# Reordered opening loads and first-chunk work in a fused attention and expert kernel

## The reference

```
B, H, S, D = 4, 8, 768, 48
for t in range(S):                                   # attention, per batch and head
    cur = einsum('bhd,bhe->bhde', u * k_t, v_t)
    y_t = einsum('bhd,bhde->bhe', r_t, state + cur)
    state = w * state + einsum('bhd,bhe->bhde', k_t, v_t)
x = y as (3072, 384)                                 # tokens x model width
h = maximum(maximum(x @ w1, x @ w2), x @ w3);  x = h @ w_out        # 384 -> 768 -> 384
logits = x @ w_gate + log1p(exp(x @ w_noise)) * noise               # 8 experts, best two
out[token] += weight * (maximum(x @ w1[e], 0) @ w2[e])              # 384 -> 1024 -> 384
```

## Time and profile before

| | before |
|---|---|
| median of 3 runs | 884.25 us |
| profiled execution | 883.62 us |
| its span | 881.7 us |
| TensorE (PE) matmul busy | 865.3 us, 98% |
| VectorE (DVE) busy | 450.2 us, 51% |
| ScalarE (ACT) busy | 270.8 us, 31% |
| GpSimd (POOL) busy | 391.4 us, 44% |

### The profile page before, as it was taken

The page is one execution under the profiler, slowest core; times in us unless marked ns, Lnnn a source line. Parts: engine busy times, 40 slices in busy tenths (PEclk is TensorE's granted clock), DMA queues, the critical chain, the costliest instruction groups (busy, mean ns, idle before and its releaser), DMA issues. The chain is left out here.

```text
span 881.7 us, 19581 instructions
## 1 busy us (share of the span) xinstructions
PE 865.3 (98%) x6562; PEld 846.8 (96%) x6563; DVE 450.2 (51%) x1100; ACT 270.8 (31%) x520; POOL 391.4 (44%) x380
## 2 busy tenths in 40 slices
PE   6999999999999999999999999999999999999996
PEld 5999999999999999999999999999999999999996
DVE  7674646546464655637574563452525335264322
ACT  4441323223231322225315342421414243143210
POOL 5254325343352544234454556453534426455442
PEclk9999999999999999999999999999999999999999
DMA  9795112222221211031115622615325252432221
GB/s 227 176 301 135 46 42 65 64 62 52 61 57 47 66 54 38 2 135 55 46 46 191 196 58 65 182 54 166 97 66 180 79 181 73 151 123 70 64 79 52
DMA packets 103765, 86.08 MB, mean 98 GB/s; under 512 B 60634, under 2 KB 93090, under 8 KB 103696
## 3 DMA queue, kind: packets, MB, share of 16 engines
q1 hardware_dynamic: 82704, 31.56, 15.1%
q10 hardware_dynamic: 8576, 27.33, 9.6%
q0 software_dynamic: 12416, 26.28, 9.5%
HBM read 70.46 MB, written 21.35 MB: 104 GB/s over the span
## 5 line engine op out<-in xcount | busy, mean ns | idle before, releaser
L1413 PE MATMUL ps<-yh,wh 128*128 128x384 f32 x432 | 148.2, 343 | 1.6 <-DVE wl L715 0.6
L1304 ACT ACTIVATE gh<-ps 128x384 fp32r<-128x384 f32 x136 | 66.9, 492 | 264.6 <-PE ps L1415 264.6
L1415 PE MATMUL ps<-yh,wl 128*128 128x384 f32 x432 | 145.1, 336 | 0.0
L1413 PE MATMUL ps<-xgh,w1h 128*128 128x384 f32 (+1 forms) x456 | 145.0, 318 | 0.0
L1414 PE MATMUL ps<-yl,wh 128*128 128x384 f32 x432 | 145.0, 336 | 0.0
L1415 PE MATMUL ps<-xgh,w1l 128*128 128x384 f32 (+1 forms) x456 | 145.0, 318 | 0.0
L1414 PE MATMUL ps<-xgl,w1h 128*128 128x384 f32 (+1 forms) x456 | 145.0, 318 | 0.0
L1060 DVE SCALAR_TENSOR_TENSOR gl<-ps,gh 128x384 fp32r<-128x384 f32 x136 | 75.8, 557 | 126.8 <-ACT gh L1304 126.8
L1413 PE MATMUL ps<-w2h,gh 128*128 128x384 f32 x408 | 138.2, 339 | 0.6 <-DVE gl L1054 0.6
L1414 PE MATMUL ps<-w2l,gh 128*128 128x384 f32 x408 | 136.6, 335 | 0.0
L1415 PE MATMUL ps<-w2h,gl 128*128 128x384 f32 x408 | 136.5, 335 | 0.0
(11 more groups left out here) (202 smaller groups left out, 1484.2 us busy)
## 6 DMA issues: line engine op xcount, KB each, us to landing
ew_raw<-ew ACTq DMA_DIRECT2D x28, 768.0 KB, 4.6
v_sb<-vN SPq DMA_DIRECT2D x24, 192.0 KB, 3.1
out<-zrow SPq DMA_DIRECT2D x1, 4608.0 KB, 15.9
x_rows<-x_sb ACTq DMA_DIRECT2D x8, 576.0 KB, 3.8
kn_sb<-kN SPq DMA_DIRECT2D x20, 192.0 KB, 2.9
k_raw<-kT SPq DMA_DIRECT2D x48, 72.0 KB, 2.3
wraw<-moe_w SPq DMA_DIRECT2D x6, 576.0 KB, 7.5
e_raw<-ew SPq DMA_DIRECT2D x4, 768.0 KB, 4.3
```

The source lines that it names most:

```text
L1304: act.activation(gh[:, f, :], ps[f % 4][:, 0:T], ACT.Relu).then_inc(gh_ok, 1)
L1413: pe.matmul(o, ah, bh, start=start, stop=False)
L1415: return pe.matmul(o, al, bh, start=False, stop=stop)
```

## The change

SyncE loads the keys of chunks 0 and 1 first, then the natural keys and values of chunk 0, then the keys of chunk 2 and, newly on SyncE, the receptances of chunk 2; the natural keys and values of chunks 1 and 2 follow. ScalarE issues the receptances of chunks 0 and 1 alone. On ScalarE k times u of chunk 0 stands ahead of `wkn`, and that of chunk 1 ahead of the copy to `wu_nat`. On TensorE the scores and the turned product of chunk 0 stand ahead of the transposes of `wkn`, and one group of four transposes by `keep_turning` is gone. The lists of VectorE and GpSimd are the same.

```diff
-            for c in range(BS):
-                load_turned(0, c)
+            load_turned(0, 0)
+            load_turned(0, 1)
+            load_keys(0, 0)
+            load_values(0, 0)
+            load_turned(0, 2)
+            sp.wait_ge(r_clear, BS)
+            for h in range(2):
+                rows, span = slice(h * HB, h * HB + HD), slice(2 * CH, 3 * CH)
+                sp.dma_start(r_raw[rows, 2, 0, :], rT[0, 2 * PAIR_OF[0] + h, :, span]).then_inc(rk_in[2], 16)
+                sp.dma_start(r_raw[rows, 2, 1:PAIRS, :],
+                             rT[0, 0:2 * PAIRS - 2].rearrange("(q h) d t -> h d q t", h=2)[h, :, :, span]).then_inc(rk_in[2], 16)
+            for c in range(1, BS):
                 load_keys(0, c)
                 load_values(0, c)
...
-            for c in range(BS):
+            for c in range(2):
                 act.wait_ge(r_clear, c + 1)
...
+            act.wait_ge(w_in, 32)
+            key_products(0)
             act.wait_ge(tab_ok, 1)
             for p in range(PAIRS):
                 ins = act.activation(wkn[:, p, :], wk[:, p, :], ACT.Copy, scale=w_dec[:, p:p + 1])
             ins.then_inc(wkn_ok, 1)
-            act.wait_ge(w_in, 32)
-            key_products(0)
+            key_products(1)
             act.wait_ge(nat_mm, 1)
             act.activation(wu_nat[:, :, :, :], ps[0][:, :].rearrange("j (q h d) -> j q h d", q=PAIRS, h=2)[:, :, :, 0:HD], ACT.Copy
                            ).then_inc(nat_ok, 1)
-            key_products(1)
             key_products(2)
...
+            products(0, 0)
+            own_sums(0, 0)
             pe.wait_ge(wkn_ok, 1)
             for p in range(PAIRS):
                 mm = pe.transpose(ps[0][:, p * P:(p + 1) * P], wkn[:, p, :], ident[:, :])
             mm.then_inc(nat_mm, 1)
-            products(0, 0)
-            keep_turning(4, 7)
-            own_sums(0, 0)
             keep_turning(3, 6)
```

## The result

The changed kernel takes 887.32 us, median of 21 runs (884.4 to 890.11). The kernel before, run beside it, takes 884.12 (883.15 to 885.52, also 21 runs). The ratio is 1.0034, with an interval of 1.0026 to 1.0043: slower, by 3.2 us, where 883.15 was forecast and the range ended at 884.8.

A forecast was written before the change was run, and what follows sets the result against it. TensorE, busy 98% of the span, was taken as the bound. `turn_wo` 1.3 us earlier, 1.2 at the first dense matmul (30.3), 1.1 kept: 883.62 becomes 882.5, predicted median 883.15, range 881.4 to 884.8.

The forecast's parts named there:

- VectorE's wait of 2.78 us: VectorE's idleness before 11.07, for ScalarE's k times u of chunk 0; forecast to fall under 1 us.
- GpSimd's 1.72 us: GpSimd's wait in the opening until chunk 1's keys were in at 11.14; forecast to be gone.
- k times u started at 8.09 instead of 7.3: ScalarE, chunk 0: four issues fewer, table load ending at 6.6, `rk_in[0]` in by 7.60 at latest; start taken as 7.3.
- The step that failed: SyncE issues `wo_raw` at about 13.5 instead of 11.66; landing between 17.0 and 18.8, taken as 17.5.
- The upper price: `wo_raw` landing if all the issue delay goes into it: 18.8, with `turn_wo` staying at 18.85.
- the queue might run dry: Transfer engines may lack work during part of the 2.0 us of small receptance issues, which carry 192 KB.
- rival A: `wo_raw` or `rk_in[2]` becomes the wait in the opening; gain 0 to 0.4 us, 884.1; chance 0.19.
- Rival C: Slow clock comes a second time, in the opening at 11.4 to 13.8; 884.75, with two stretches 886.4; chance 0.09.
- Rival B: Slow clock at the dense stage's start goes as work comes earlier; gain 2.8 us together, 881.45; chance 0.20.
- the premise that once the first dense matmul has begun nothing else binds: Dense stage: other engines' steps are hidden unless they stop TensorE; only how early the first dense matmul begins counts.

The follow-up runs named there:

- r2_on_act: The changed kernel with chunk 2's receptances issued by ScalarE again, SyncE's four issues for them gone; 893.0 us, ratio 0.9994 to the kernel before.
- loads_only: The kernel before with only the change's new order of loads, compute in the old order; 892.82 us, ratio 1.0036.
- r2_on_sp: The kernel before with only chunk 2's receptances moved to SyncE, behind that chunk's keys; 894.9 us, ratio 1.0015.
- order_only: The kernel before with only the change's compute order on ScalarE and TensorE, loads as before; 892.98 us, ratio 0.9995.
- wo_early: The changed kernel with both `wo_raw` transfers issued ahead of chunk 2's natural keys and values, receptances still on SyncE; 891.79 us, ratio 1.0022.
- order_warm: The kernel before with the change's compute order and six identity transposes behind the last `fold`; 883.25 us, ratio 0.9984.
- warm_short: The changed kernel with 16 identity transposes ahead of `turn_wo`, in the wait for `wo_raw`; 894.89 us, ratio 1.0031 to the kernel before.
- warm_wait_again: The changed kernel with 28 identity transposes ahead of `turn_wo`, in the wait for `wo_raw`, a repeat; 886.71 us, ratio 1.0024 to the kernel before.
- order_again: Repeat of the kernel before with only the change's compute order, loads as before; 893.42 us, ratio 1.0002.
- before_warm: The kernel before with only six identity transposes added behind the last `fold`; 891.84 us, ratio 0.9989.
- r2act_warm: The changed kernel with chunk 2's receptances back on ScalarE and six identity transposes behind the last `fold`; 892.05 us, ratio 0.9979 to the kernel before.

## Why the prediction was wrong

**What held.** VectorE's wait of 2.78 us shrank to 0.91, with r times ku taken at 9.40 beside the forecast 9.42, and `q_hat` of chunk 1 ended at 11.85 (11.65). GpSimd's 1.72 us is gone, its two `k_hat` run from 7.79 to 11.30 (11.1). `wu_nat` came at 11.89 and `k_upd` at 12.46 (12.0 and 12.5), chunk 1's masks ended at 16.89 (17.0). All that was worked out on engines was right within about 0.2 us. And in `r2_on_act`, where nothing holds `turn_wo`, the first dense matmul is at 30.49, forecast 30.3. One miss is on ScalarE: k times u started at 8.09 instead of 7.3.

```profile
6.79 1.28 ACT L1271 ACT_TABLE_LOAD   x1 [6.66 <-DMA k_raw<-kT]
8.09 1.28 ACT L1271 ACTIVATE rku<-k_raw,u_sb 128x128 f32<-128x128 f32 x4
```

The table load did not start at 5.3, when ScalarE had issued its last transfer, but behind the wait for chunk 0's keys. That 9.40 met the forecast 9.42 is luck: the forecast let VectorE wait for the end of `k_hat`, and the trace names ScalarE's product, which ended at 9.37, while `k_hat` ran to 9.5 or later. Whether the late product cost anything is not shown.

**The step that failed** is SyncE's: "I take a quarter of the delay: 17.5". The issue was placed well (13.5, measured 13.27). The landing was priced between 17.0 and 18.8 and came at 20.3, beyond both ends. The upper price assumed that a transfer issued 1.8 us later lands at most 1.8 us later. That holds only if as much has been moved by then as before. It hadn't: 0.53 MB less had been moved by 16 us, worth 1.6 us. From 16 us to the landing 0.42 MB passed in the kernel before (1 us at 415 GB/s) and 1.48 MB in the changed one (345 GB/s to 18, 344 to 20.3). That is 1.06 MB, or 3.1 us, more: the 0.53 MB that were behind, and as much again that went by ahead of `wo_raw` or beside it. This is bookkeeping, and it gives 3.1 of the 3.3 us. The loads ahead of `wo_raw` are the same in both kernels, so the second half can only be of transfers issued behind it (the second `wo_raw` and the first `wraw`), which share the transfer engines with it; why they took more of them this time is not shown. The sentence that the queue might run dry for part of the 2.0 us was right, and it should have been followed with the numbers at hand: 192 KB in four issues of 0.5 us are 98 GB/s, against the 180 of the earlier trace rows.

So it was rival A in mechanism, with its price too low: the forecast of A let `turn_wo` start at 18.8 at worst, and so had no loss at all in it. Nor did any term hold what came on top in the profiled execution, the fall of the clock while TensorE stood (1.68 + 0.69 us) and `wl` behind `k_hat` (0.82). Runs show that the four issues are the cause of the wait: the wait appears with the issues on SyncE in the changed kernel (2.76 and 1.94 us), in `loads_only` (2.00) and in `r2_on_sp` (1.22), and is absent without them (`r2_on_act`, `order_only`). The ratio follows in `r2_on_act` (0.9994) and `loads_only` (1.0036). That the wait is the whole price is not shown, since `wo_early` has no wait and still 1.0022.

**The rule of the Trainium skill**, DMA: Bandwidth & Descriptors (Issuing engines are not separate DMA queues), that issuing from several engines saves only sequencer time, usually small beside the transfer, is what spoke for putting all on SyncE. Here the trace disagrees with the second half of it: with transfers of 24 and 72 KB the sequencer's time was the limit, 108 GB/s against 232, and `r2_on_act`, which gives four issues back to the other engine, has 195 and no wait.

**The clock.** Rival C had a second fall in the opening at 11.4 to 13.8, where TensorE has four transposes less. There it did not come. It came in the wait for `wo_raw`, in one of the changed kernel's two profiles, and cost 1.68 + 0.69 us there. C's worst, 886.4, is the case nearest to the result, for another reason than it gave.

**Rival B** held that an earlier start would let the dense work escape the slow stretch. `r2_on_act` starts at 30.49 and has it all the same (about 31.1 to 34.5). An earlier start did not remove it. Six transposes ahead of the dense stage went with a higher mean clock, but no run shows what decides on it in a single execution. And the premise that once the first dense matmul has begun nothing else binds was false by 1.2 us in `order_warm`: with an earlier start and full clock VectorE's chain to `hmax` stops TensorE.

**Open.** How much of the loss is the clock's. `warm_short` and `warm_wait_again` have no better mean clock than the changed kernel, though in their profiles it stays at 1.00 through the wait. Falls elsewhere are on record: `warm_short` has one from 33.7 to 37.1 and one from 460 to 464, `loads_only` one from 83 to 86, `order_again` one from 81 to 88. How often they come in the runs without a profile is not known. Why `wo_early` is slower. Why the level differs by up to 9 us between sets: every profile of the slower sets but that of `r2_on_sp` has a stall of 1.5 to 3.5 us without a releaser ahead of the `y_n` transposes that start between 81 and 85 us, those of 884 us have none there, and the falls from 81 us on begin in such a stall or shortly behind it. The kernel before was not profiled on the slow level, so whether it has them too is known only from `before_warm` (2.00 us). Here is that of `r2act_warm`:

```profile
PE ps L1412 <- issue: 3.4, 1, 3.4
```

## What to carry to other kernels

Before moving a small load to a queue, divide its bytes by the time of an issue there. If that rate is below what the transfer engines move, as here (98 GB/s against 180 to 232), the load can leave them idle, and a large transfer behind it can be late by more than the issues themselves: here 1.6 us of issuing became 3.3 us at the landing. Here it helped to give the small loads to a second issuing engine. To put the large load ahead of them took the wait away and not the lost time.

An earlier start of the bounding engine is worth only what its next supplier can follow. And where the granted clock is low at the start of the bounding engine's long stage, a few cheap instructions ahead of it are worth a try: kernels with six transposes there came to 0.9984, 0.9979 and 0.9989 (the last with an interval that reaches 1.0002), and the gain went with the clock.

## What the runs showed of the hardware

- From one issue on SyncE's queue to the next it took 0.46 to 0.55 us in the changed kernel's opening whatever the size, 24, 192 or 576 KB; the kernel before has one of 0.85 (the gates, at 10.81). Eight issues of 24 and 72 KB hold the queue at about 102 GB/s.
- The same program waits 2.76 us in one execution and 1.94 in another for the same load. With the first the granted clock fell to 0.50 after the engine had stood since 17.55, with the second it stayed at 1.00.
- The granted clock also fell to 0.50 while TensorE was at work: at 29.1 inside the last `fold` matmuls (`order_only`), at 30.5 as six transposes began (`before_warm`).
- At 1.2 GHz 18 transposes took 4.10 us, at 2.4 GHz 2.38.
- ScalarE's table load stood behind the semaphore wait of the first activation: 6.79 instead of 5.3.
- VectorE's `wl`, 1.35 us at 30.03 before GpSimd's `k_hat` began (30.95), took 2.17 when it started 0.3 us behind GpSimd's `k_hat` (33.85 beside 33.55), 0.82 us more.
